# Two of the sixteen blocks of w3 times w_out multiplied in plain fp32, in place of fillers, and the rest of that product one step sooner

## What is computed

```
out_d    = sm_attn(q_d, k_d, v_d)            # q, k, v averaged over groups of 4 tokens
out_local = softmax(mask(|i-j| < 4) of q k^T / 8) @ v
x  = repeat(out_d, 4) + out_local            # laid out as 2304 x 512
x2 = ((x @ w1) * (x @ w2)) @ w3 @ w_out      # w1, w2: 512 x 1024; w3: 1024 x 1024; w_out: 1024 x 512
out = silu(x2 @ w_in) @ w_out2               # w_in: 512 x 2048
```

## Time and profile before

| | us |
|---|---|
| median of 3 runs | 798.93 (798.71 to 800.37) |
| the profiled execution, its own time | 798.51 |
| its span, first to last instruction | 796.5 |
| TensorE clock granted over the span | 1.000 of full |
| PE busy | 780.6 |
| DVE busy | 592.4 |

### The profile page before, as it was taken

One profiled execution on the slowest core, in us unless ns is written; L12 is line 12 of the kernel. 1 busy time (PEld: TensorE's weight loads), 2 busy tenths in 40 slices (PEclk: granted clock), 3 DMA queues, 4 the chain that ended last, 5 costly groups with the idle time before them and its releaser, 6 DMA issues.

```text
span 796.5 us, 13873 instructions
## 1 busy us (share of the span) xinstructions
PE 780.6 (98%) x5386; PEld 695.5 (87%) x5386; DVE 592.4 (74%) x943; ACT 346.5 (43%) x791; POOL 271.8 (34%) x301
## 2 busy tenths in 40 slices
PE   8899999999999999999999999999999999999997
PEld 5678778899998999999999998898898988889996
DVE  6998989866667767677698767778677679676644
ACT  6989886333433235323354332363233244322321
POOL 7888885433133221423313211303131113112000
PEclk9999999999999999999999999999999999999999
DMA  9867721201101111110123112213221122322002
GB/s 316 262 225 246 244 92 47 74 28 53 53 27 54 53 35 46 53 49 32 53 80 107 54 53 78 81 54 132 83 76 54 56 89 94 108 68 91 27 0 80
DMA packets 23041, 69.84 MB, mean 88 GB/s; under 512 B 2496, under 2 KB 2496, under 8 KB 22976
## 3 DMA queue, kind: packets, MB, share of 16 engines
q1 hardware_dynamic: 22976, 68.95, 26.7%
HBM read 64.23 MB, written 4.72 MB: 87 GB/s over the span
## 4 chain that ended last, share of the span: by engine, by line
PE 88%; DVE 8%; issue 1%; ACT 1%; POOL 1%; DMA 0%; DVEq 0%; POOLq 0%
PE ps L1051 44%; PE ps L1109 25%; PE ps L1080 13%; PE ps L1131 3%; DVE qkd L761 1%; DVE sc L773 1%; DVE r L833 1%; DVE low L781 1%; DVE x L815 1%; PE ps L1210 1%; PE ps L1152 1%; DVE wa L719 1%; PE ps L1197 1%; DVE tr L713 1%; PE ps L1167 0%
## 5 line engine op out<-in xcount | busy, mean ns | idle before, releaser
L1051 PE MATMUL ps<-xb,wa 128*128 128x384 f32 x2016 | 404.9, 338 | 0.6 <-DVE mu L879 0.5
L1051 PEld LDWEIGHTS ps<-xb,wa 128*128 128x128 f32 x2016 | 355.0, 188 | 22.6 <-DVE mu L879 1.5
L381 POOL TENSOR_TENSOR rw<-rw 128x256 f32<-128x256 f32 x188 | 167.5, 911 | 447.3 <-DMA rw<-in_sets 336.0
L879 DVE TENSOR_TENSOR mu<-ps,mu 128x384 f32<-128x384 f32 x132 | 73.1, 554 | 122.0 <-PE ps L1051 121.8
L1080 PE MATMUL ps<-g,r 128*128 128x512 f32 (+1 forms) x576 | 124.9, 338 | 1.9 <-issue 1.9
L613 ACT ACTIVATE a<-a 128x384 f32<-128x384 f32 x72 | 37.9, 527 | 188.9 <-DVE a L879 188.9
L1109 PE MATMUL ps<-w2h_even,g 128*128 128x512 f32 x432 | 113.2, 394 | 0.0
L1109 PE MATMUL ps<-w2h_odd,g 128*128 128x512 f32 x432 | 112.5, 393 | 0.0
L719 DVE TENSOR_TENSOR wa<-rw,wa 128x1024 fp32r<-128x1024 f32 x96 | 107.1, 1116 | 3.3 <-ACT wa L445 3.2
L1080 PEld LDWEIGHTS ps<-g,r 128*128 128x128 f32 x576 | 97.7, 188 | 10.4 <-issue 2.5
L1109 PEld LDWEIGHTS ps<-w2h_odd,g 128*128 128x128 f32 x432 | 79.9, 188 | 11.9
(11 more groups left out here) (79 smaller groups left out, 703.1 us busy)
## 6 DMA issues: line engine op xcount, KB each, us to landing
rw<-in_sets SPq DMA_DIRECT2D x48, 512.0 KB, 3.5
w2r<-in_w_out SPq DMA_DIRECT2D x24, 512.0 KB, 3.5
qk<-in_qk SPq DMA_DIRECT2D x16, 576.0 KB, 6.0
vg<-in_vg SPq DMA_DIRECT2D x16, 336.0 KB, 4.6
vw<-in_vw SPq DMA_DIRECT2D x16, 320.0 KB, 3.4
out<-osb SPq DMA_DIRECT2D x18, 256.0 KB, 2.1
wn<-in_w SPq DMA_DIRECT2D x16, 256.0 KB, 4.6
raw<-in_w_out SPq DMA_DIRECT2D x2, 1024.0 KB, 8.8
```

Source lines behind the costliest of these rows:

```text
L381: nc.gpsimd.tensor_tensor(blocks[:, o, :], blocks[:, a, :], blocks[:, b, :], op).then_inc(done, 1)
L879: nc.vector.tensor_tensor(o, half_bank(k, i), term, ALU.add).then_inc(sum_ready, 1)
L1051: e = nc.tensor.matmul(ps[:, (k + i) % 2, 0:TH], wa[:, k % 2, l, A_SLOT[i], a * P:(a + 1) * P], xb[:, i, r, a, :], start=(i in (0, 1, 4) a ...
```

## The change

In words: halves 0 and 1 are no longer split into high and low parts. `multiply(q < RAW = 2)` takes the raw w3 from `wn` and the raw w_out from `raw3` and issues one plain fp32 matmul of 512 columns for each part. Part 0 of half 0 stands in step 2 and its parts 1 to 3 in step 3, at places where fillers stood. Half 1 takes step 4, and from there each half stands one step sooner (`FOLD` is 3). Step 16 has three halves. The low part of a w_out block may only be written once the fp32 matmul has read the raw data (`raw_used`), so all low parts of w_out move one step later, and the high parts are dealt out anew. In step 16 ACT and DVE have one `w3_high` and one `w3_low` less.

```diff
@@ constants
-        FOLD = 4
+        FOLD = 3
-        W_OUT = {1: (0, 1), 2: (2, 3), 3: (4, 5), 4: (6, 7)}
+        HIGHS = {1: (0,), 2: (1, 2), 3: (3,), 4: (4, 5, 6), 5: (7,)}
+        LOWS = {3: (0, 1), 4: (2, 3), 5: (4, 5), 6: (6, 7)}
-        FILL = {1: (15, 2, 1), 2: (3, 3, 1), 3: (3, 3, 1)}
+        FILL = {1: (15, 2, 1), 2: (3, 0, 0)}
+        SOON = {2: ((), (0,), ()), 3: ((1,), (2,), (3,))}
+        RAW = 2
         def halves_of(s):
-            return range(max(s - FOLD, 0), s - FOLD + 1 if s < PAIRS else HALVES)
+            return range(max(s - FOLD, 1), s - FOLD + 1 if s < PAIRS else HALVES)
         def splits_of(s):
-            return range(max(s - FOLD + 1, 0), s - FOLD + 2 if s < PAIRS else HALVES)
+            return range(max(s - FOLD + 1, RAW), s - FOLD + 2 if s < PAIRS else HALVES)
@@ SP
             def load_w3(q):
-                after(sp, w3_lo, q - 1)
+                if q < 2 * RAW:
+                    after(sp, w3_mul, q - 1)
+                else:
+                    sp.wait_ge(w3_lo, q - 1 - RAW)
@@ ACT, last step
-                    w3_high(HALVES - 3)
+                    w3_high(HALVES - 2)
                     first_weights_high(0)
                     first_weights_high(1)
                     copy_pt()
                     copy_ptd()
+                    w3_high(HALVES - 1)
+                    take_w3o(MT - 2)
@@ DVE
-                for n in W_OUT.get(s - 1, ()):
+                for n in LOWS.get(s, ()):
                     dve.wait_ge(r3_hi, n + 1)
+                    if n % (MT // 2) < 3:
+                        dve.wait_ge(raw_used, 3 * (n // (MT // 2)) + n % (MT // 2) + 1)
+                    else:
+                        dve.wait_ge(w3_mul, n // (MT // 2) + 1)
...
-                if s == PAIRS - 1:
-                    take_w3o(MT - 3)
...
-            w3_low(HALVES - 3)
+            w3_low(HALVES - 2)
             weights_low(0, 0)
-            w3_low(HALVES - 2)
             weights_low(0, 1)
+            w3_low(HALVES - 1)
@@ PE
+                if q < RAW:
+                    if part == 0:
+                        pe.wait_ge(w3_here[q], 16)
+                        pe.wait_ge(r3_in[q], 16)
+                    e = nc.tensor.matmul(ps[:, fold_bank(q), :], wn[:, q, part * P:(part + 1) * P], raw3[:, a, BANK:],
+                                         start=a == 0, stop=a == MT - 1)
+                def between(n):
+                    if s in FILL:
+                        warm(FILL[s][n])
+                    for part in SOON[s][n] if s in SOON else ():
+                        multiply(0, part)
```

More of the change, by code:

```diff
@@ L186, in attention_then_mlps @@
             sem("w3_hi"), sem("w3_lo"), sem("w3_mul"), sem("w3o_hi"), sem("w3o_lo"))
-        r3_hi, r3_lo = sem("r3_hi"), sem("r3_lo")
+        r3_hi, r3_lo, raw_used = sem("r3_hi"), sem("r3_lo"), sem("raw_used")
         tr_ready, xb_hi, xb_lo = sem("tr_ready"), sem("xb_hi"), [sem(f"xb_lo{n}") for n in range(7)]
@@ L318, in _ @@
                     load_qk(3)
+                    load_w3(0)
                 if t + 1 < PAIRS:
                     load_vg(t + 1)
-                if t >= FOLD - 2:
+                if t > 1:
                     load_w3(t - FOLD + 2)
@@ L390, in w3_low @@
             def w3_low(q):
-                pool.wait_ge(w3_hi, q + 1)
+                pool.wait_ge(w3_hi, q + 1 - RAW)
                 m4 = slice(4 * (q % 2), 4 * (q % 2) + 4)
@@ L546, in step @@
                     act.wait_ge(pooled, PAIRS)
-                    w3_high(HALVES - 2)
                     tokens_high(0, 0)
@@ L552, in step @@
                     take_down()
-                    w3_high(HALVES - 1)
-                    take_w3o(MT - 2)
-                    act.wait_ge(w3_lo, HALVES)
+                    act.wait_ge(w3_lo, HALVES - RAW)
                     tokens_high(0, 3)
@@ L575, in step @@
                     exps_down()
+                if s == PAIRS - 1:
+                    exps_down()
                 for q in halves_of(s):
@@ L578, in step @@
                         take_w3o(q // 2)
-                if s == PAIRS - 1:
-                    exps_down()
                 if 0 < s < FOLD:
                     take_down()
-                for n in W_OUT.get(s, ()):
+                for n in HIGHS.get(s, ()):
                     act.wait_ge(r3_in[n // (MT // 2)], 16)
@@ L750, in w3_low @@
             def w3_low(q):
-                dve.wait_ge(w3_hi, q + 1)
+                dve.wait_ge(w3_hi, q + 1 - RAW)
                 m4 = slice(4 * (q % 2), 4 * (q % 2) + 4)
@@ L856, in _ @@
             take_local(PAIRS - 2)
[L857 to L858 removed]
+            dve.wait_ge(w3_lo, HALVES - RAW - 2)
+            w3_low(HALVES - 2)
             dve.wait_ge(wa_first, 1)
             weights_low(0, 0)
[L861 removed]
             dve.wait_ge(wa_hi, 1)
             weights_low(0, 1)
+            w3_low(HALVES - 1)
             tokens_low(0, 0)
@@ L1118, in multiply @@
                 m, a = q // 2, 4 * (q % 2) + part
-                if part == 0:
-                    pe.wait_ge(w3_hi, q + 1)
-                    pe.wait_ge(w3_lo, q + 1)
-                    if q % 2 == 0:
-                        if m == MT - 1:
-                            pe.wait_ge(exp_d, PAIRS)
-                        else:
-                            after(pe, w3o_lo, m)
-                if q < 2:
-                    n = MT // 2 * q + part
-                    pe.wait_ge(r3_lo, n + 1)
-                for p, (l, r) in enumerate(((0, 0), (1, 0), (0, 1))):
-                    e = nc.tensor.matmul(ps[:, fold_bank(q), :], w3t[:, l, a, :], r3[:, a, r, :],
-                                         start=(a == 0 and p == 0), stop=(a == MT - 1 and p == 2))
+                if q < RAW:
[4 more added lines that the diff above has]
+                                         start=a == 0, stop=a == MT - 1)
+                else:
+                    if part == 0:
+                        pe.wait_ge(w3_hi, q + 1 - RAW)
+                        pe.wait_ge(w3_lo, q + 1 - RAW)
+                        if q % 2 == 0:
+                            if m == MT - 1:
+                                pe.wait_ge(exp_d, PAIRS)
+                            else:
+                                pe.wait_ge(w3o_lo, m)
+                    if q < 2 + RAW:
+                        pe.wait_ge(r3_lo, a + 1)
+                    for p, (l, r) in enumerate(((0, 0), (1, 0), (0, 1))):
+                        e = nc.tensor.matmul(ps[:, fold_bank(q), :], w3t[:, l, a, :], r3[:, a, r, :],
+                                             start=(a == 0 and p == 0), stop=(a == MT - 1 and p == 2))
                 if part == 3:
                     e.then_inc(w3_mul, 1)
+                elif q < RAW:
+                    e.then_inc(raw_used, 1)
             def warm(n):
@@ L1231, in step @@
                     return
-                soon = s > FOLD and s + 1 < PAIRS
                 whole = s > FOLD + 1
-                if soon and whole:
+                soon = whole and s + 1 < PAIRS
+                def between(n):
[3 more added lines that the diff above has]
+                        multiply(0, part)
+                if soon:
                     scores_local(s + 1)
-                warm(FILL[s][0] if s in FILL else 0)
+                between(0)
                 scores_down()
-                if soon and not whole:
-                    scores_local(s + 1)
                 for part in range(0 if whole else 2):
@@ L1245, in step @@
                     turn_local()
-                    warm(FILL[s][1] if s in FILL else 0)
+                    between(1)
                     turn_down()
-                    warm(FILL[s][2] if s in FILL else 0)
+                    between(2)
                 for part in range(0 if whole else 2, 4):
```

3 lines of the change are left out of this document (removed).

## The result

| | before | changed |
|---|---|---|
| median | 799.62 us (798.71 to 800.37, 4 runs) | 794.29 us (793.97 to 794.59, 4 runs) |
| the profiled execution, its own time | 798.51 | 793.97 |
| its span | 796.5 | 792.1 |
| end of the last copy that DVE makes | 792.82 | 789.57 |

The ratio is 0.9934, with a 95% interval of 0.9921 to 0.9948: faster by 0.66%. The forecast was 796.9 with a range down to 795.0, so the direction was right, and more was won than it said. Between the two profiled executions 4.54 us lie, of which the engines' work explains 792.82 - 789.57 = 3.25.

The account below looks back on a forecast made before the run. PE (98% busy) counts overall, but early the chain runs through DVE in steps 2 to 6 and 12 to 14 and the end of step 16. Product 3 moves from 134.93 to 132.9: -2.0 us, median 796.9, range 795.0 to 799.0.

Parts of the forecast that it names:

- The fp32 product (0.86): Step 2 on PE: one fp32 product takes 0.86 us against 0.64 for the filler it replaces, +0.21.
- `max_down(3)` (25.25): Step 2 and head of step 3: `max_down(3)` starts at 25.25 instead of 25.89, -0.64 us.
- a sign of being wrong: Signs against the forecast included fp32 products over 1.05 us apart and `turn_down(7)` at or before 56.5.
- Steps 3 to 6 on DVE, +1.1: Pairs of low parts at 2.11 us put `turn_down(7)` at 57.63 instead of 56.52: +1.1, step 2's gain included.
- The waits that are added: Steps 2 to 5: new waits for `raw_used` and for w3 loads cost nothing on the chain.
- Steps 12 to 14, -0.68: DVE's chain there holds one `take_w3o` instead of two, so 0.68 us is won.
- Step 16: PE takes 11.2 us instead of 14.79; DVE, one low part less, ends its add at 132.9, when product 3 starts.
- the ends of 0.61 and 1.74: Bounds in us on what DVE saves by one low part of w3 less in step 16; 1.2 was taken.
- Sum: All places together: product 3 starts at 132.9 instead of 134.93, -2.0 us.
- The likeliest case: The forecast itself, chance 0.52: 1.2 to 3.0 us won, 795.9 to 797.7.
- The second rival, cheap subtractions: Steps 3 to 6, chance 0.16: two or three pairs cost 1.28, not 2.10; 3.0 to 4.3 us won.
- The sum against the time: From 798.51, the profiled execution's own time, to 796.5; the median lies 0.42 higher, at 796.9.

Follow-up runs that it names:

- before_a: The kernel before, unchanged, run once more for a second trace: that execution took 799.70 us instead of 798.51.
- w3o_later: The changed kernel with `take_w3o` behind `max_down` in DVE's queue instead of ahead of it: 796.74 us, ratio to before 0.9965.
- fold4: The changed kernel's fp32 halves 0 and 1, but in steps 4 and 5, with all fillers and four halves in step 16: 798.81 us, ratio to before 0.9990.
- more_dve: The changed kernel with one more low-part subtraction on DVE in step 16, its result unread: 794.48 us, ratio to before 0.9940.
- exps_wait: The changed kernel with step 15's pooled exponentials on ACT waiting again for the finished half: 795.22 us, ratio to before 0.9954.
- before_low2: The kernel before with step 2's pair of low parts moved behind `pool_pair`: 798.64 us, ratio to before 0.9991.
- before_sp: The kernel before with twelve more waits, on a value long reached, in SP's queue: 799.52 us, ratio to before 1.0005.
- fillers: The changed kernel with 11 filler units put back beside the fp32 products of steps 2 and 3: 797.04 us, ratio to before 0.9971.

## Why the prediction was right and wrong

- **The fp32 product (0.86) and `max_down(3)` (25.25).** Right: 25.36, and 0.86 for two of the products of steps 2 and 3. The one ahead of `scores_down(3)` took 1.06, over the 1.05 that was named as a sign of being wrong. It did no harm, since the filler at the same place had taken 0.84 and not the 0.64 that was charged for it: the difference is the +0.21 of the sum.
- **Steps 3 to 6 on DVE, +1.1.** Wrong by 1.2 us: `turn_down(7)` stands at 56.44, not 57.63, and so below the 56.5 that was named as a sign of being wrong. The form of the sum holds, since from `max_down(6)` it is 8.47 as from its pattern, 8.45. The spacings were mis-sized: 7.04, 8.36 and 7.21 against 7.91, 8.5 and 7.52. I had carried each pair at 2.11. Step 3's cost 1.28, and POOL's sum beside it 2.41, where the kernel before had 2.18 and 1.45; step 5's cost 1.89. ACT's lateness in step 4 was 0.16 and not 0.3. The rule of the Trainium skill that the prediction weighed (SBUF — State Buffer, "SBUF: two separate sides") is that whoever starts first holds the shared pair for a whole instruction. The lengths fit it: in step 3 POOL's sum took 1.41 more than its 1.00, beside a pair of 1.28, and in step 2 of before_a the pair took 1.16 more than its 1.28, beside sums of POOL. Who starts first can't be checked in the records, where POOL's start stands 0.27 ahead of DVE's in step 3, and POOL waited all the same:

```profile
25.77 2.41 POOL L414 TENSOR_TENSOR vt<-vg 112x384 f32<-112x384 f32 x1
```

  My own rows had both prices, and I moved the pairs by 0.6 without asking again which would hold.
- **The waits that are added: nothing.** Right. No L846 waited, and ACT took half 2's raw data in step 4 at 33.82 with no wait for the load.
- **Steps 12 to 14, -0.68.** Wrong in the path: nothing was won, `turn_down(15)` is at 111.89 and was at 111.96. One `take_w3o` did leave, but the pace doesn't hang on it. The profile's chain names it, since it goes back along DVE's instructions and doesn't show that one of them was held up by POOL. Each of these steps has a token sum on DVE (L713 before, L722 now), and beside it POOL makes a low part of w3. Step 14 before, then changed:

```profile
107.12 1.34 DVE L713 TENSOR_TENSOR tr<-x 128x768 f32<-128x768 f32 x1
106.35 1.29 POOL L393 TENSOR_TENSOR w3t<-wn,w3t 128x512 fp32r<-128x512 f32 x1
...
106.44 1.94 DVE L722 TENSOR_TENSOR tr<-x 128x768 f32<-128x768 f32 x1
106.28 1.30 POOL L403 TENSOR_TENSOR w3t<-wn,w3t 128x512 fp32r<-128x512 f32 x1
```

  DVE reached the sum 0.68 sooner, and the sum took 0.60 longer. In all six cases, three steps in either kernel, it ends 0.80 to 0.82 us after POOL's low part, whenever DVE comes to it. From there DVE's mask and minima release POOL's queue for the next round, so from step 13 on the round runs through POOL, 7.28 us from step to step in both kernels, and `take_w3o`, `max_down` and `pool_pair` have slack beside it. This is read from the traces. No run was made for it, but the step is 7.27 to 7.29 us in w3o_later too, where `take_w3o` stands behind `max_down`, and in fold4, where it stands in the steps of before.
- **Step 16.** PE's side is exact: 11.18 us against 11.2. DVE's side was mis-sized: 13.72 us of work, where 15.8 - 1.2 = 14.6 was said. The low parts of w3 cost 1.00 + 1.22, and had cost 1.82, 1.22 and 0.68: 1.5 less, inside the ends of 0.61 and 1.74. But the prediction gave this to the low part that is gone, and more_dve, which has three again, takes only 0.24 more: its three cost 0.99, 1.22 and 0.68. What made the first one cheap is that POOL starts its division sooner (116.61, not 118.11), since the copy of a half no longer holds ACT up. exps_wait shows it: with that release undone the first low part costs 1.83. The tokens' low parts cost 5.78 instead of 6.45 in all, which the prediction hadn't seen: POOL's own `xb` waits 1.63 for ACT and comes later, so that DVE's first ran in 0.95 instead of 1.76.
- **Sum.** -2.0 was said. On the engines it was -3.25: -1.2 from the early pairs, +0.7 for steps 12 to 14, and -0.9 from DVE's work in step 16 make -1.4 of difference, which meets the 1.33 by which product 3 came earlier than 132.9. The likeliest case had two of its three places right (step 16 and the early pairs, not steps 12 to 14). The second rival, cheap subtractions, had the right size, in part by luck: one early pair of four came at the low price, and it had counted on two or three.
- **The sum against the time.** This is the step that took the result out of the range. "Behind it DVE and PE go on as before" put what follows the last copy at nothing. It measured 1.3 us between the profiled executions: 1.1 behind the copy, and 0.2 outside the span. With -3.25 on the engines alone the median would have been 798.93 - 3.25 = 795.7, inside the range; with the other 1.3 it comes to 794.4, and 794.29 was measured. Why the end is shorter stays open.
- **The gain against the medians.** Against 799.62, the median of before with one more run, the gain reads 5.3 us: 3.25 on the engines, 1.3 behind them, and 0.8 because the profiled execution of before lies 1.11 under that median, and that of the changed kernel 0.32 under its own. The profiled one of before has the low price in step 2, and many of its runs seem to have the high one. That makes the gain larger, but has no part in the miss of the time.

No variant ran faster than the changed kernel by more than the measurement tells.

## What to carry over

Where the profile shows two prices for one instruction beside the same neighbour, don't extrapolate either price from step to step: let both outcomes into the range at each place, since the records' starts don't tell who will wait. Before an instruction's time is booked as won, check that the round to the next step really runs through it; here a sum beside POOL took the gain up. Before a forecast is made against a median, look at a second trace of the same kernel, since one may be of the rarer kind. In the last stage before a change of phase ask for every engine that bounds it what shortens it; here PE lost a half, and DVE got shorter mostly because POOL was out of its way sooner.

## What was unexpected of the hardware

- In two executions of the same kernel, with starts that agree within 0.02 us, DVE's pair of step 2 took 1.28 or 2.44 and POOL's sum 2.26 or 1.00. The last copy, 770 us later, ended 1.3 us apart (792.82 and 794.14).
- The last 1.1 us between the kernels are not on any engine: the wait for the last store's landing was 1.7 in before, before_a, before_low2 and before_sp, and 0.6 in the changed kernel and all of its variants. A fetch of instructions falls beside it in the first. Lengthening three engines' queues moved the fetch and 0.6 us of the end, but not the time. The cause stays open.
- The 15 units of fillers of step 1 took 3.49 us in the traced execution of before, 4.00 in before_a, 4.48 in the changed kernel and 4.83 in fillers, at the same granted clock of 1.000. The trace gives no reason, and the slack in front of the next wait mostly took it up.
- An fp32 product of 512 columns took 0.86 to 1.06 us, and the three fp32r matmuls that stand for it 2.98 / 4 = 0.75. So on PE plain fp32 is 15% to 40% dearer here, and it saves ACT, DVE and POOL the splitting. The Trainium skill, FP8 and Floating Point Precision, "TensorE Precision Notes", says that true fp32 takes four passes through the array. The trace fits this, if one fp32r matmul is one pass: 0.86 is 3.5 times, and 1.06 is 4.3 times, the 0.25 of one (2.98 / 12).
